# RWKV-style attention and two expert layers in one program: a second tile with an empty slot, keys and receptance loaded on waits of their own, one level's products in other banks, 48-channel states

## What is computed

```python
for t in range(S):
    cur = np.einsum('bhd,bhe->bhde', u[None] * kt, vt)
    y[:, :, t] = np.einsum('bhd,bhde->bhe', rt, state + cur)
    state = wt[:, :, :, None] * state + np.einsum('bhd,bhe->bhde', kt, vt)
...
x = y.transpose(0, 2, 1, 3).reshape(B * S, H * D)          # 3072 x 384
h = x @ w_in;  g = where(h >= 1, h, where(h <= -1, 0, (h + 1) ** 2 / 4));        x = g @ w_out
h = x @ w2_in; g = where(h > 0, h, exp(min(h, 0)) - 1);                          out = g @ w2_out
```

## Time and profile before

| | us |
|---|---|
| median of three runs (985.79 to 989.73) | 988.8 |
| the profiled execution's own time | 988.76 |
| its span, first to last instruction | 986.9 |
| TensorE busy in the span | 975.1 |
| VectorE busy | 589.6 |
| ScalarE busy | 502.4 |
| GpSimd busy | 48.5 |

### The profile page before, as it was taken

One profiled execution on the slowest core, in us unless ns is written; L12 is line 12 of the kernel. 1 busy time (PEld: TensorE's weight loads), 2 busy tenths in 40 slices (PEclk: granted clock), 3 DMA queues, 4 the chain that ended last, 5 costly groups with the idle time before them and its releaser, 6 DMA issues.

```text
span 986.9 us, 22374 instructions
## 1 busy us (share of the span) xinstructions
PE 975.1 (99%) x9722; PEld 800.3 (81%) x9722; DVE 589.6 (60%) x919; ACT 502.4 (51%) x896; POOL 48.5 (5%) x44
## 2 busy tenths in 40 slices
PE   8999999999999999999999999999999999999998
PEld 6899897888888788888888888888888888888886
DVE  7798878888888788878344645333333334333332
ACT  3665545354544535453556766455445544444443
POOL 6930000000000000000000000000000000000000
PEclk9999999999999999999999999999999999999999
DMA  9732312022220222112050000000000000000000
GB/s 320 239 117 88 115 73 91 3 98 81 98 81 2 90 89 81 55 61 98 1 193 33 33 33 0 33 33 1 33 33 33 31 2 33 33 1 0 33 1 33
DMA packets 24833, 61.67 MB, mean 62 GB/s; under 512 B 2464, under 2 KB 7200, under 8 KB 24736
## 3 DMA queue, kind: packets, MB, share of 16 engines
q1 hardware_dynamic: 24736, 60.25, 17.2%
HBM read 50.80 MB, written 9.44 MB: 61 GB/s over the span
## 4 chain that ended last, share of the span: by engine, by line
PE 94%; DVE 4%; DMA 1%; issue 1%; ACT 0%; SPq 0%; ACTq 0%; DVEq 0%
PE down_banks L701 41%; PE work_banks L701 29%; PE first_up_bank L701 22%; DVE att L1268 2%; PE work_banks L816 1%; PE work_banks L896 1%; DMA att<-kT_dram 1%; DMA att<-wT_dram 1%; DVE att L1280 0%; DVE g_lo L1431 0%; DVE work_banks L1280 0%; DVE att L1250 0%; DVE work_banks L1455 0%; DVE ynat L1393 0%; DVE ynat L1390 0%
## 5 line engine op out<-in xcount | busy, mean ns | idle before, releaser
L701 PE MATMUL down_banks<-g_hi,wout_lo 128*128 128x512 f32 (+1 forms) x624 | 244.6, 392 | 0.1
L701 PE MATMUL down_banks<-g_hi,wout_hi 128*128 128x512 f32 (+1 forms) x624 | 235.6, 378 | 0.0
L701 PE MATMUL down_banks<-g_lo,wout_hi 128*128 128x512 f32 (+1 forms) x624 | 235.0, 377 | 0.0
L1431 DVE TENSOR_TENSOR g_lo<-scratch,g_hi 128x512 fp32r<-128x512 f32 (+1 forms) x192 | 128.1, 667 | 111.9 <-ACT g_hi L1019 111.6
L1019 ACT CAST g_hi<-scratch 128x512 fp32r<-128x512 f32 (+1 forms) x192 | 116.0, 604 | 98.1 <-PE down_banks L701 72.5
L1119 ACT ACTIVATE scratch<-first_up_bank,consts 128x512 f32<-128x512 f32 (+1 forms) x88 | 57.2, 650 | 194.6 <-PE first_up_bank L701 108.4
L701 PEld LDWEIGHTS down_banks<-g_hi,wout_lo 128*128 128x128 f32 x624 | 117.4, 188 | 27.0 <-DVE g_lo L1431 0.8
L701 PEld LDWEIGHTS down_banks<-g_hi,wout_hi 128*128 128x128 f32 x624 | 117.3, 188 | 23.7
L701 PEld LDWEIGHTS down_banks<-g_lo,wout_hi 128*128 128x128 f32 x624 | 117.6, 188 | 20.7
L1532 DVE SCALAR_TENSOR_TENSOR scratch<-scratch,work_banks 128x512 f32<-128x512 f32 x72 | 49.5, 687 | 133.2 <-ACT scratch L1191 133.2
L701 PE MATMUL first_up_bank<-x_hi,win_lo 128*128 128x512 f32 (+1 forms) x336 | 127.9, 381 | 0.4 <-DVE x_lo L1436 0.2
(11 more groups left out here) (128 smaller groups left out, 1142.3 us busy)
## 6 DMA issues: line engine op xcount, KB each, us to landing
att<-rT_dram SPq DMA_DIRECT2D x12, 512.0 KB, 3.6
att<-kT_dram SPq DMA_DIRECT2D x12, 512.0 KB, 4.5
att<-wT_dram SPq DMA_DIRECT2D x12, 512.0 KB, 5.7
r_nat<-rN_dram SPq DMA_DIRECT2D x12, 384.0 KB, 4.5
k_nat<-kN_dram SPq DMA_DIRECT2D x12, 384.0 KB, 4.8
att<-vN_dram SPq DMA_DIRECT2D x12, 384.0 KB, 5.7
x_dram<-r_nat SPq DMA_DIRECT2D x18, 256.0 KB, 2.3
ynat<-x_dram SPq DMA_DIRECT2D x6, 768.0 KB, 4.2
```

The source lines that it names most:

```text
L701: return nc.tensor.matmul(out, lhsT, rhs, start=start, stop=stop, **kw)
L1431: nc.vector.tensor_tensor(g_of(g_lo, F), sum_of(F), g_of(g_hi, F).bitcast(F32), ALU.subtract).then_inc(glo_ready, 1)
```

## The change

Five edits that touch tiles 0 and 1 and one that touches all states.

1. `load_group(2, 0)` issues keys and receptance before its wait for the states, the keys behind `kt_filled` (the keys before have been transposed, slot 19), the receptance behind `y_filled` (the rows before are done, slot 19). The order becomes keys, receptance, decays, values.
2. The products of level 1 of (0, 1) go to `down_banks`, so they don't wait for the mask of level 0 any more. `down(0)`, the first to write there, waits for the mask of level 1. In slot 0 VectorE updates before it masks.
3. WORK_TILE_1: slot 33 is empty; the last level of (2, 0) moves to 34, the first pair of (2, 1) to 35, `turn_k` and `row_0` share slot 36, and the second pair, `row_1` and the third pair follow in 37, 38 and 39. `attend` of chunks 2 to 5 doesn't wait for the copied keys.
4. In slot 32 `lo_of_g(31)` stands behind the first masked copy and `sum_with_q(32)` ahead of the update of the keys; both were at the end.
5. `bonus` and `sums` of (2, 1) move from slots 38 and 39 to slot 33, `values` of (2, 0) from 36 to 34.
6. `state_step` uses 48 stationary columns instead of 64, `from_state` 48 rows instead of 64.

The diff, cut to its core:

```diff
-WORK_TILE_1 = {0: [("pair", 0, 0, 4)], 1: [("last", 0, 0)], 2: [("pair", 0, 1, 0)], 3: [("turn_k", 0, 0)],
-               4: [("pair", 0, 1, 2)], 5: [("row_0", 0, 0)], 6: [("pair", 0, 1, 4)], 7: [("row_1", 0, 0)],
-               8: [("last", 0, 1), ("turn_x", 0, 0)]}
+WORK_TILE_1 = {0: [("pair", 0, 0, 4)], 2: [("last", 0, 0)], 3: [("pair", 0, 1, 0)], 4: [("turn_k", 0, 0), ("row_0", 0, 0)],
+               5: [("pair", 0, 1, 2)], 6: [("row_1", 0, 0)], 7: [("pair", 0, 1, 4)], 8: [("last", 0, 1), ("turn_x", 0, 0)]}
...
-DIAGONAL_TILE_1 = {4: [("values", 1, 0)], 6: [("bonus", 1, 1)], 7: [("sums", 1, 1)], 8: [("values", 1, 1), ("keys", 2, 0)],
+DIAGONAL_TILE_1 = {1: [("bonus", 1, 1), ("sums", 1, 1)], 2: [("values", 1, 0)], 8: [("values", 1, 1), ("keys", 2, 0)],
...
         def product_banks(k, g, l):
-            return down_banks[:, 0:2, :] if (k, g) == (0, 0) and l % 2 else g_banks[:, :, :]
+            return down_banks[:, 0:2, :] if (k, g) == (0, 0) and l % 2 or (k, g, l) == (0, 1, 1) else g_banks[:, :, :]
...
             def load_group(k, g):
+                inputs = (kT, k_, rk_in), (rT, r_, rk_in), (wT, w_, w_in), (vN, v_, v_in)
+                if (k, g) == (2, 0):
+                    sp.wait_ge(kt_filled, B + 2)
+                    sp.dma_start(k_[g], kT[k, g]).then_inc(rk_in[g], 16)
+                    sp.wait_ge(y_filled, 3 * (B + 2))
+                    sp.dma_start(r_[g], rT[k, g]).then_inc(rk_in[g], 16)
+                    inputs = inputs[2:]
                 sp.wait_ge(state_ready, k * B - 2 + 2 * g)
-                for src, dst, done in ((rT, r_, rk_in), (kT, k_, rk_in), (wT, w_, w_in), (vN, v_, v_in)):
+                for src, dst, done in inputs:
...
             def pair_products(k, g, l):
-                if (k, g) != (0, 0) and (k < 2 or l < NL - 1):
+                if (k, g) != (0, 0) and (k, g, l) != (0, 1, 1) and (k < 2 or l < NL - 1):
...
             def attend(k, b):
-                if k > 0 or b >= 2:
+                if k == 1 or k == 0 and b >= 2:
                     pe.wait_ge(kt_copied, k * B + b + 1)
...
                 def from_state(i, a, h):
-                    ps, j = slice(a * PAD, (a + 1) * PAD), (b % 2) * HP + i
+                    ps, j = slice(a * PAD, a * PAD + D), (b % 2) * HP + i
...
             def state_step(k, b):
-                        last = mm(banks(k, b)[2][a * PAD:(a + 1) * PAD, i * D:(i + 1) * D],
-                                  k_turned(k, b)[:, i * P + a * PAD:i * P + (a + 1) * PAD],
+                        last = mm(banks(k, b)[2][a * PAD:a * PAD + D, i * D:(i + 1) * D],
+                                  k_turned(k, b)[:, i * P + a * PAD:i * P + a * PAD + D],
...
             def down(F, tiles=range(KT)):
                     pe.wait_ge(glo_ready, F + 1)
+                    if F == 0:
+                        pe.wait_ge(masked[1], masked_after(0, 1, ("level", 1)))
...
             def pair_slot(F, k, g, l):
                     nc.vector.copy_predicated(scores[:, :, :, m:4 * m], adjacent_mask, adjacent).then_inc(masked[g], 1)
+                if F == FIRST[1]:
+                    lo_of_g(F - 1)
...
                 if l < 4:
                     lo_of_g(F - 1)
+                if l < 4 or F == FIRST[1]:
                     sum_with_q(F)
...
                 if l < 4:
                     ahead_of(k, g, l + 2)
-                else:
+                elif F != FIRST[1]:
                     lo_of_g(F - 1)
                     sum_with_q(F)
...
             def first_tile_slot(F):
-                if level is not None:
+                if level is not None and F > 0:
                     mask(*level)
                 if F in SUM_AHEAD:
                     sum_with_q(F)
                 if level is not None:
                     update(*level)
+                if F == 0:
+                    mask(*level)
```

More of the change, by code:

```diff
@@ L355, in work_at @@
                 return []
-            table = WORK_TILE_1 if c == 1 and f in WORK_TILE_1 else WORK
-            return [(what, c + 1 + ahead_, *rest) for what, ahead_, *rest in table[f] if c + 1 + ahead_ < NC]
+            table = WORK_TILE_1 if c == 1 and f <= max(WORK_TILE_1) else WORK
+            return [(what, c + 1 + ahead_, *rest) for what, ahead_, *rest in table.get(f, []) if c + 1 + ahead_ < NC]
         def diagonal_at(F):
@@ L1238, in mask @@
                     dve.wait_ge(scores_zeroed[g], 1)
+                if (k, g, l) == (0, 1, 1):
+                    dve.wait_ge(masked[g], masked_after(0, 1, ("level", 0)))
                 products = product_banks(k, g, l).rearrange("p a (j t) -> p (a j) t", t=PAD)[:, :, 0:HALF // 2]
@@ L1489, in layer1_slot @@
                 work = work_at(F)
-                before = [what for what, *_ in work_at(F - 1)]
-                for what, k, g, *l in work_at(F - 1):
-                    if what == "pair" and l[0] < 4 and before == ["pair"] and not work[0][0].startswith("row"):
-                        suffixes(k, g, l[0] + 2)
                 if work and work[0][0] == "pair":
@@ L1502, in layer1_slot @@
                 for what, k, g, *l in work_at(F - 1):
-                    if what == "pair" and l[0] < 4 and work[0][0].startswith("row"):
+                    if what == "pair" and l[0] < 4:
                         suffixes(k, g, l[0] + 2)
```

## The result

The changed kernel takes 985.83 us (median of 22 runs, 983.37 to 989.80), the kernel before beside it 988.22 us (22 runs, 985.55 to 990.85). The ratio is 0.9971 with a 95% interval of 0.9961 to 0.9982: 2.9 us less, between 1.8 and 3.9. The forecast was 985.0 in a range of 981.8 to 987.8, and a change within 0.5%. The profiled execution of the changed kernel took 986.49 us.

The account below looks back on a forecast made before the run. TensorE, busy 975.1 of 986.9 us, was taken as the bound. Savings of 1.1 (load), 0 (banks), 0.4 (table), 0 (shared slot 36, third pair) and 2.3 (states) gave 3.8 off 988.76: 985.0 us, range 981.8 to 987.8.

Parts of the forecast that it names:

- the 1.6 us at the down banks: TensorE's wait for the update in the first slots; one of two pieces, 1.4 us, was placed before slot 0.
- the 0.73 us of the earlier trace: TensorE's wait before level 1 of (0, 1) in slot 1, at 34.59 us; the upper bound of that gain.
- Rival 5: Another condition, such as the last masks of (1, 1), holds level 0 of (2, 0); 986.1 us, chance 0.04.
- The bound of the loss, 0.3 us: Largest loss allowed for level 1 of (0, 1) in the down banks, from slot 1's waits moved apart.
- rival 3: More comes back: slot 1's wait 0.7 us, the start of tile 1 1.0, the states 2.6; 983.3 us, chance 0.18.
- the two new waits: Start of tile 1: 0.4 us before `up(34)` for ScalarE's reads, 0.35 us before `down(32)` for `lo_of_g(32)`.
- Rival 4: VectorE becomes the bound in slots 33 to 36, losing 5.5 us if all is exposed twice; 990.9 us, chance 0.06.
- the narrow margin in slot 40: Last level follows the third pair after 4.35 us; VectorE needs 3.9, so it fits by some 0.3 us.
- the chain without gaps: Sign against the prediction: VectorE busy without gaps through slots 33 to 40.
- Rival 1: In the states, a 48-column load takes as long as one of 64; 987.3 us, chance 0.17.
- Rival 2: Full-height state instructions have a pace floor between 22.9 and 29.4 ns, taken at 26; 986.1 us, chance 0.08.
- the second half: The program's unchanged second half; another length there would show the prediction wrong.

Follow-up runs that it names:

- x_loads: Kernel before with only the early load of keys and receptance of (2, 0); ratio to the kernel before 0.9979 (0.9962 to 0.9995).
- x_banks: Kernel before with only level 1 of (0, 1) in the down banks and slot 0 updating before masking; ratio 1.0000 (0.9982 to 1.0019).
- v_before: The kernel before, unchanged, run and profiled once more; 987.55 us.
- y_keys_41: Changed kernel with the keys step of (3, 0) moved from slot 40 to slot 41, behind the last update; 986.57 us, ratio to the kernel before 0.9973.
- x_states: Kernel before with only 48 stationary columns in the state products and 48 rows in the state reads; ratio 0.9985 (0.9964 to 1.0005).
- z_state_sizes: Changed kernel with state products 32 x 48 in odd batches, 48 x 32 in even ones; runs of 16 took 0.53 and 0.55 us, against 0.56.

## Why the prediction was right, point by point

**The bound.** TensorE's sum was the right frame: every part of the gain is a stretch in which TensorE has less to do or waits less. One row was misread. Both pieces of the 1.6 us at the down banks lie before slot 0 (0.16 us at 8.30 and 1.39 at 15.32); the wait of slot 1 is in another row of that list, for the work banks. As the sum used the 0.73 us of the earlier trace rows, nothing hung on it.

**Edit 1: 1.1 us forecast, 1.9 measured on the average.** The wait went wholly, as forecast, and nothing else was late. The mis-sized term is the wait as the measure of the load's cost. The one profiled execution had 1.17 us, others 0 to 1.26; and the traffic of four loads at once cost about another microsecond, 0.75 of it in gaps named "issue", in which TensorE waits for its own instructions. I had left them out. The upper bound of 1.2 was too low. Rival 5 is excluded, since x_loads alone moved the start of level 0.

**Edit 2: 0 forecast, 0 or a loss of 0.8.** The reason given was right: VectorE has no gap from slot 0 to 3, so a reordering gains nothing there, and the stretch took 9.61 us with it (x_banks) and without it (v_before). The bound of the loss, 0.3 us, was too small. The earlier trace rows held the clue, the update of 2.07 us; I read it in rival 3 as something that another order could undo, when it was something that another order could just as well bring. This half of rival 3 fell.

**Edits 3 and 4: 0.4 forecast, 0.37 measured, with a wrong account.** Of the two new waits the first came as said (0.29 us for 0.4), the second, 0.35 us before `down(32)`, did not: VectorE was ahead. So the start gained 0.7 us. The 0.3 that came back did so in slot 41, which was in none of my steps: I had followed the shared slot 36 and the third pair, and called 35 to 40 free by comparing work, without following the keys step that now stands ahead of the last update and of `x_lo`. Two errors of a third of a microsecond cancelled, which was luck. Rival 4 is excluded: `up(32)` to `up(38)` is shorter.

**Edit 5: 0 forecast.** Slots 38 to 40 show no new wait; the narrow margin in slot 40 held. VectorE has gaps of 1.4 and 2.2 us in slots 37 and 39, so the chain without gaps that would have spoken against the prediction isn't there. With y_keys_41 slots 38 to 42 take 23.32 us, as in x_states.

**Edit 6: 2.3 us forecast, 1.9 measured behind slot 22 and 0.4 more by estimate.** The size of one instruction was met: (0.92 - 0.23) / 31 = 22.3 ns against 22.9 forecast and 29.4 before, the load's record 124 ns against 122. 352 of them at 7.1 ns would be 2.5 us; in the stretches 6.5 ns of these arrive. Rival 1 would have left the run at 1.14 us. Rival 2 is excluded as well: it would have held the pace between 22.9 and 29.4 ns, and it is 22.3. That is below the 25 ns that the Trainium skill gives as a floor ("TensorE: Matmul & The Clock Gate", "Back-to-back issue gap"), here for two tiles of full height. The reason, though, was only half right: z_state_sizes shows that the moving side would have stopped the gain at about this size. `from_state` changed nothing, as forecast, 133 ns a load before and after.

**The sum.** By the stretches: 1.9 to 2.3 for the states, 1.9 for the load, 0.37 for the table, and 5/7 x 0.8 = 0.6 lost in slot 1, 3.6 to 4.0 us together. From `up(0)` to `up(104)` the two pairs of executions differ by 4.2 and 3.2 us, 3.7 on the average. The timed runs have 2.9 with an interval to 3.9. The forecast of 3.8 and its 985.0 are met within the interval, but in part by luck: the load was too low by 0.8, slot 1 too high by 0.6, and the second half, of which the prediction said that another length there would prove it wrong, is 1.1 us longer on the average in the executions with 48 columns. That may be scatter, as said above; if it isn't, it is a loss that stood in none of the forecast's steps, and it could be what separates 3.7 from 2.9. Rival 3, at 983.3, would have needed the whole 0.7 of slot 1, of which nothing came, and 1.0 us at the start of tile 1, where 0.7 came.

## What to carry to other kernels

A wait in one profiled execution measures neither its mean nor the whole of what its cause costs: profile the same kernel twice, and look in the slots behind it for gaps named "issue" and for the instruction packet ahead of each. When a step is moved past another, follow every step of the list that moves with it to its own reader, also where the work per slot seems the same. Before an instruction of VectorE with two SBUF inputs is moved, look at what GpSimd runs at that time and which of the two would start first.

## What the runs showed of the hardware

**The clock dips early, in some executions.** v_after, the same program as the changed kernel, took 1.93 and 2.50 us for its first runs:

```profile
5.58 1.93 PE L707 MATMUL work_banks<-att 64*64 64x32 f32 x64
7.45 2.50 PE L707 MATMUL work_banks<-x_lo 128*128 128x512 f32 x5
```

The kernel before took 1.14 and 1.43 us for the same. Each further one of the five matmuls took (2.50 - 0.50) / 4 = 0.50 us in place of 0.23, about twice as long, until about 11 us. That would fit the lower of TensorE's two levels, 1.2 GHz instead of 2.4, but the granted clock reads 1.00 there, so it is argued and not shown. x_loads did the same. In the changed kernel the slow stretch is at 16.88 us, and there the granted clock shows it, with 0.50. `up(0)` started at 29.7 to 30.2 us in the five executions without edit 1 and at 29.9 to 33.1 in the nine with it. The two sets hardly overlap, so an effect of the edit, or of the longer program, is neither shown nor excluded; nothing in the trace ties it to the edit. Of the 22 timed runs of the changed kernel 9 have a mean clock below 1.000 (median 987.1, the others 985.0), and of the 35 of the kernel before beside the single parts 20 (989.6 against 987.9). It is a scatter of 2 us, as large as the larger terms of the sum.

**TensorE waits for its instructions.** They come in packets of 16 KB, 77 for this program, and the first matmul of a new packet never started less than 1.24 us behind the packet's end. Where the large loads went out together, such a packet started later: in slot 24 that cost 0.2 to 1.2 us in five of six executions.

**Small tiled matmuls** go at 22.3 ns for 48 x 48 at full height, about 21 for 32 x 48 and 48 x 32, and a change of the tile's width cost about 0.1 us in the one row that shows it.

**Loads of 512 KB**: the keys took 3.9 to 4.5 us from issue to landing when they went early, with little beside them, and 5.3 to 6.6 us as the second of four loads issued at once. The receptance, first of the four, took 3.9 to 4.2 even then.
